# Numerators of full tiles and the turned sums over ones, each product taken as two column halves of 64

## The reference, cut to what matters

```python
# B, H, S, D = 4, 8, 576, 64; w_phi is 64 x 128
def phi(x):
    proj = einsum('bhsd,df->bhsf', x, w_phi)
    proj = proj - max(abs(proj), axis=-1, keepdims=True)
    return concatenate([exp(proj), exp(-proj)], axis=-1)
q_p, k_p = phi(q), phi(k)
kv  = einsum('bhsf,bhsd->bhfd', k_p, v)
z   = sum(k_p, axis=2)
num = einsum('bhsf,bhfd->bhsd', q_p, kv)
den = einsum('bhsf,bhf->bhs', q_p, z)[..., None] + 1e-06
attn = num / den
```

## Time and profile before

| | us |
|---|---|
| median of three runs | 910.85 (910.55 to 911.68) |
| the profiled execution | 910.34 |
| its span, first to last instruction | 908.7 |
| TensorE busy | 886.8 (98%) |
| VectorE busy | 432.3 (48%) |
| ScalarE busy | 293.9 (32%) |
| GpSimd busy | 123.4 (14%) |
| granted TensorE clock | 0.999 of full speed |

### The profile page before, as it was taken

The page is one execution under the profiler, slowest core; times in us unless marked ns, Lnnn a source line. Parts: engine busy times, 40 slices in busy tenths (PEclk is TensorE's granted clock), DMA queues, the critical chain, the costliest instruction groups (busy, mean ns, idle before and its releaser), DMA issues.

```text
span 908.7 us, 15622 instructions
## 1 busy us (share of the span) xinstructions
PE 886.8 (98%) x5888; PEld 811.7 (89%) x5889; DVE 432.3 (48%) x875; ACT 293.9 (32%) x479; POOL 123.4 (14%) x145
## 2 busy tenths in 40 slices
PE   8999999999999999999999999999999999999996
PEld 6795968779999999999988999999999999999996
DVE  5678687898767644333457422222222222222222
ACT  4545454572155532223353321121112112112111
POOL 1010302122344112222300010010001001001001
PEclk9999999999999999999999999999999999999999
DMA  9513713112457432346743630030020002000000
GB/s 296 178 54 124 271 52 104 53 48 59 157 177 196 79 58 71 26 78 122 159 157 114 181 112 1 1 105 1 0 70 35 0 2 102 0 0 35 1 1 35
DMA packets 37181, 75.31 MB, mean 83 GB/s; under 512 B 8176, under 2 KB 24688, under 8 KB 35472
## 3 DMA queue, kind: packets, MB, share of 16 engines
q1 hardware_dynamic: 32832, 56.07, 23.2%
q0 software_dynamic: 3488, 17.85, 5.3%
q10 hardware_dynamic: 816, 0.79, 0.3%
HBM read 51.06 MB, written 23.64 MB: 82 GB/s over the span
## 4 chain that ended last, share of the span: by engine, by line
PE 89%; DVE 5%; issue 2%; ACT 2%; DMA 1%; POOL 0%; POOLq 0%; DVEq 0%; SPq 0%; ACTq 0%
PE ps L1023 10%; PE ps L1025 10%; PE ps L1024 10%; PE ps L822 6%; PE ps L1038 5%; PE ps L1039 5%; PE ps L1037 5%; PE ps L925 4%; PE ps L938 3%; PE ps L926 3%; PE ps L927 3%; PE ps L940 3%; PE ps L939 3%; PE ps L769 3%; PE ps L729 2%
## 5 line engine op out<-in xcount | busy, mean ns | idle before, releaser
L1023 PE MATMUL ps<-xnH,blkH 128*128 128x384 f32 x576 | 193.7, 336 | 3.0 <-DVE blkL L1690 1.9
L1025 PE MATMUL ps<-xnH,blkL 128*128 128x384 f32 x576 | 193.4, 336 | 0.0
L1024 PE MATMUL ps<-xnL,blkH 128*128 128x384 f32 x576 | 193.2, 335 | 0.0
L1697 DVE TENSOR_TENSOR sg<-sg,ps 128x384 f32<-128x384 f32 x72 | 39.8, 553 | 245.5 <-ACT sg L1256 241.6
L1256 ACT ACTIVATE sg<-ps 128x384 f32<-128x384 f32 x72 | 35.4, 491 | 252.1 <-PE ps L1025 252.1
L1023 PEld LDWEIGHTS ps<-xnH,blkH 128*128 128x128 f32 x576 | 108.2, 188 | 7.5 <-issue 4.3
L1024 PEld LDWEIGHTS ps<-xnL,blkH 128*128 128x128 f32 x576 | 108.2, 188 | 2.6
L1025 PEld LDWEIGHTS ps<-xnH,blkL 128*128 128x128 f32 x576 | 108.1, 188 | 0.0
L1038 PE MATMUL ps<-blkL,hH 128*128 128x512 f32 x216 | 84.8, 393 | 0.0
L1039 PE MATMUL ps<-blkH,hL 128*128 128x512 f32 x216 | 84.8, 392 | 0.0
L1037 PE MATMUL ps<-blkH,hH 128*128 128x512 f32 x216 | 84.5, 391 | 0.0
(11 more groups left out here) (219 smaller groups left out, 1593.6 us busy)
## 6 DMA issues: line engine op xcount, KB each, us to landing
stage<-in_ffn_w SPq DMA_DIRECT2D x12, 768.0 KB, 4.3
xin<-xs_dram SPq DMA_DIRECT2D x9, 578.2 KB, 9.9
xs_dram<-zrow SPq DMA_DIRECT2D x8, 578.2 KB, 8.6
qT<-in_q SPq DMA_DIRECT2D x4, 1152.0 KB, 5.5
xnH_dram<-xoH SPq DMA_DIRECT2D x8, 576.0 KB, 3.5
xnL_dram<-xoL SPq DMA_DIRECT2D x8, 576.0 KB, 6.1
xnH<-xnH_dram SPq DMA_DIRECT2D x6, 768.0 KB, 5.4
xnL<-xnL_dram SPq DMA_DIRECT2D x6, 768.0 KB, 6.3
```

The costliest lines, as they stand in the source:

```text
L1023: e.matmul(o, hi, xnH[par][:, c, :], start=(c == 0), stop=False)
L1024: e.matmul(o, hi, xnL[par][:, c, :], start=False, stop=False)
L1025: last = e.matmul(o, lo, xnH[par][:, c, :], start=False, stop=(c == KC - 1))
```

## The change

A full tile's product of a head and sign, 128 stationary columns, becomes two products of 64 stationary columns each, g = 0 and g = 1, with the same 81 moving columns. They write partitions 0 to 63 and 64 to 127 of the same PSUM columns. The four products of the turned sums over ones become eight in the same way. Order, waits and semaphores stay, and no other engine's instructions change.

```diff
@@ -791,8 +791,9 @@
                     if c == 1:
                         for i in range(4):
-                            last = e.matmul(ps[:, TURNED[1], ZC + i * KC:ZC + (i + 1) * KC], zT[:, i, :], zsel[:, :],
-                                            start=True, stop=True)
+                            for g in range(2):
+                                last = e.matmul(ps[rows_half(g), TURNED[1], ZC + i * KC:ZC + (i + 1) * KC],
+                                                zT[:, i, rows_half(g)], zsel[:, :], start=True, stop=True)
                         last.then_inc(s["pe_C"], 1)
@@ -819,8 +820,10 @@
                 for h in range(half * 4, half * 4 + 4):
                     for sign in range(2):
-                        last = e.matmul(num_of(at)[0:n, h // 4, h % 4, :], ex[:, at[1] % 2, sign, h, 0:n],
-                                        kvs[:, h // 2, sign * 2 + h % 2, :], start=(sign == 0), stop=(sign == 1))
+                        for g in range(2):
+                            last = e.matmul(num_of(at)[rows_half(g), h // 4, h % 4, :],
+                                            ex[:, at[1] % 2, sign, h, rows_half(g)],
+                                            kvs[:, h // 2, sign * 2 + h % 2, :], start=(sign == 0), stop=(sign == 1))
                 if half == 1:
                     last.then_inc(s["pe_N"], 1)
```

## The result

The changed kernel takes 904.36 us in the median (902.82 to 906.22, five runs) against 910.85 (909.9 to 911.68, five runs): a ratio of 0.9933, 95% interval 0.992 to 0.9947. It is faster, but the gain is 6.5 us where 11.5 were forecast. The profiled execution took 903.42 us, with a span of 901.8 and a granted TensorE clock of 0.999. The five runs spread by 3.4 us, and the spread goes with the clock: 902.82 and 903.42 at 0.999, 904.36 at 0.997, 906.21 and 906.22 at 0.994.

What follows compares the result with a forecast made beforehand. TensorE bounds the kernel, with VectorE close behind in attention. Gains of 9.33 us (three batches), 2.17 (last batch) and 0 (turned sums) sum to 11.5: 898.8 against the profiled execution, 899.3 as median; range 896.2 to 904.5.

Steps and rivals of the forecast that it cites:

- The price of a full product: TensorE's numerators: a full product as two halves costs 0.143 us instead of 0.22, from the packed tile's 0.071 per product.
- the rival of half gain: Full-tile numerators: halves reading the same 81 columns cost 0.014 us more per half product, giving 904.4 us; chance 0.11.
- The prediction's own sign: Numerators on TensorE: a block of 32 records lasting over 1.6 us would mean that the pairing costs.
- The prices of the blocks: Numerators in slots 7, 8, 9, 0: savings 0.95 per long block, 0.31 short, 0.57 slot 8's second half; 3.40 us a batch.
- The entry from the transposes: Three blocks entered from L849: 0.09 us extra each assumed, as from L731 (0.21 instead of 0.12).
- The turned sums: TensorE's sums over ones, 8 records becoming 16: taken as 0, bounds -0.7 to +1.3 us for four batches.
- VectorE's limit: VectorE's idle time in attention caps the gain at 3.11 us in each of three batches and 2.17 in the last.
- The last batch: Attention's end: VectorE also splits weights, its idle times of 0.56, 0.99 and 0.62 allowing 2.17 us.
- a new idle time in slots 2 to 4: Sign that the prediction is wrong: idle time there that takes the shift back.
- The slower rival: Numerators: column halves do not overlap, a full product still costs 0.22 us and gaps remain; 918.8 us, chance 0.05.
- The rival at the tail: First expert's rows end as late as now, losing the last batch's 2.17 us: 901.5; chance within the forecast's 0.83.

Runs made afterwards that it cites:

- turn_only: Kernel before the change with only the turned sums in column halves, numerators whole; 909.66 us, ratio 1.0002.
- before_early_scatter: Kernel before the change with the last routing step in slot 5 instead of 6, so the scatter is issued earlier; 913.2 us, ratio 1.0035.
- late_scatter: Changed kernel with one wait on GpSimd, so the loop's scatter starts only after slot 7's numerators; 909.9 us, ratio 1.0005.
- halves_in_turn: Changed kernel with earlier routing and scatter, each block taking all products of columns 0 to 63, then all of 64 to 127; 922.76 us.
- plain_aside: late_scatter plus five plain transfers of the same rows from GpSimd's queue in slot 7, where the scatter stood; 911.57 us, one run.
- full_later_padded: slot7_full_later with 64 semaphore instructions in an untaken branch of TensorE's program, shifting the code behind attention; 900.91 us, ratio 0.9904.
- before_late_scatter: Kernel before the change with the GpSimd wait that starts the scatter only after slot 7's numerators; 911.88 us, ratio 1.0027.
- slot7_full_later: Changed kernel with slot 7's tile kept in full 128-column products in batches 1 to 3, halved in batch 0; 905.18 us, ratio 0.995.

## Why the prediction was right and wrong

**The price of a full product** (0.143 us instead of 0.22) held: 64 records take 2.40 us where nothing disturbs them, 32 take 1.34. The two halves of a full tile read the same 81 columns at once, and that costs nothing; the rival of half gain, which rested on that cost, is out, although its 904.4 us is nearly the time measured. The right time came from another mechanism, and that the measured time lies inside the stated range at all, which was stretched to 904.5 for the sake of this rival, is luck. The prediction's own sign tells the two apart: a block of 32 above 1.6 us would have been the pairing.

**The prices of the blocks** held to 0.03 us: long 2.83 (forecast 2.86), short 1.70 (1.72), the second half of slot 8 1.39 (1.39). The entry from the transposes cost 0.20, as assumed.

**The turned sums** were put at nothing and gained 0.5 us in the trace, within the bounds; turn_only cannot tell it from nothing.

**VectorE's limit** was the right kind of bound and its size slightly low: with the scatter moved on both sides the gains were 3.7, 3.2, 3.2 and 3.1 us against 3.11 three times and 2.17. The last batch gave 0.9 more than its idle times allowed by my count, but that stretch has a lower clock in both profiles. The medians differ by 11.0, less than these 13.2 together; the profiled executions differ by 12.3, since the one of before_early_scatter was 1.9 us slower than its median.

**The step that failed** is that nothing else stands in the way of a block: the prediction took a duration measured with 16 and 32 records in slot 1 and put it into slot 7, and never asked what other engines do in slot 7. From L731 to the second record behind, where 2.86 us were forecast and 0.95 saved against 3.81, slot 7 took 4.97, 5.12 and 4.82 us in batches 1 to 3, so it lost 1.0 to 1.3 instead. There GpSimd issues the five indirect transfers of the batch before. While it does, TensorE gets about five records in 0.72 us (late_scatter), and the three long blocks took 6.4 us more than forecast. The kernel before gave no sign, since the earlier trace rows show its records going at their own pace beside the same transfers. What could have warned stands in GpSimd's timeline, which was not among the four views: the same five transfers, from 91.43 to 97.83. I had listed "a new idle time in slots 2 to 4" as what would prove me wrong; it came in slot 7.

**The slower rival** did not come, and halves_in_turn shows what it would have cost. The Trainium skill, "TensorE: Matmul & The Clock Gate", Part 3, "What overlaps and what doesn't", ties the overlap of weight loads with matmuls to different row groups. The rows here disagree: both halves use all rows, their loads take 136 ns each, and 64 of them pass in 2.40 us, one each 36 ns, as long as their columns alternate.

**The rival at the tail** (the gain given back to the first expert's rows) came in part: TensorE now waits 2.47 us for them. But the rows came earlier too, since scatter and loading moved forward with attention: GpSimd began to gate them at 211.07 instead of 217.08 and was done at 214.14 instead of 219.11. From the last turn to the first expert product the kernel gained 0.44 us, and its slot 7 lost 1.99 in that stretch; together 2.4, against 2.17 forecast.

**The sum by its steps:** 11.5 forecast, and the four stretches, with what their slot 7 lost put back, gave 3.68, 3.63, 3.97 and 2.43, 13.7 in all, 2.2 more than forecast. Less 6.4 in slot 7 that is 7.3, which is how far TensorE came forward between the first turn and the first expert product. Of it 6.9 are left at the end of the span and 6.5 in the medians, some of whose runs had a lower clock.

**What stays open** is why indirect transfers on GpSimd hold TensorE up. That it is the supply of its instructions is my reading of "issue"; no row shows it, and the late signals, which also strike full products, may be the same disturbance or another. plain_aside rules out the bytes and the share of the DMA engines; late_scatter rules out the place in the program and the operands. Why late_scatter and plain_aside spared batch 3 is not known. Plain transfers issued beside such a block, or other kinds of GpSimd instruction, were not tried, nor was the changed kernel with the padding alone, so how much of full_later_padded's lead is due to the full blocks and how much to the new addresses is not settled beyond the one stall of 3.74 us.

## What to carry to other kernels

A change that replaces few long instructions with many short ones raises the rate at which an engine must be fed. Before taking the price of such a block from one place in the program to another, look at what every other engine issues beside the new place, even where it shares no data, and above all for indirect transfers on GpSimd. Where a part of a change lands in such a place, leaving that part out can beat doing all of it: here the long form in one slot of three batches, with the code behind it shifted, ran 3.9 us faster than the whole change on the same chip. And moving the transfers away from the block was not free either: they cost 2.4 and 3.7 us in their new places even with full products.

## What the runs showed of the hardware

- While GpSimd issued indirect transfers (0.91 to 1.15 us each, 0.3 us apart), TensorE's records of the numerators came five in 0.72 us; undisturbed, 64 of them pass in 2.40. In batch 3 of late_scatter and plain_aside a block of 32 beside them was spared. With the DMA engines 0.98 busy at 356 GB/s from plain transfers already issued, nothing of the kind happened.
- Beside the same issuing, other engines took up TensorE's results late: 2.5 us after the products' end in before_late_scatter, with full products, where the kernel before has 0.04.
- Two products of 64 columns in the two column halves cost 0.036 us a record when they alternate and 0.060 when they do not; one of 128 columns costs 0.111.
- In late_scatter TensorE was busy for 2.03 of the 4 us from 150, and the granted clock of the next four was 0.62; in slot7_full_later it stood for 3.74 us, and the clock from 673.6 to 677.0 was 0.50, the lower of its two levels, 1.2 GHz. The changed kernel's first profile has blocks of 4.4 to 4.7 us with the same gaps and no lower clock behind them.
- The same FFN code stood for 3.74 us in one profile and not at all in another with 64 untaken instructions ahead of it; the queue marked as instruction had 41 packets in the first and 32 in the second.
- GpSimd's gating of the first expert's rows took 3.07 us for three tiles where it had taken 2.03; VectorE's splitting of weights (L1453, 1.77 us) lay wholly beside it, where before only its first 0.75 us did.
